# A third buffer for one pair of q and k loads, in the still empty weight slot of the sixth unit, and that unit's rounding three slots later

## The reference

```python
# attention inside chunks of 64 tokens
scores = q_c @ k_c.T / 8
attn = exp(scores - max(scores));  attn = attn / (sum(attn) + 1e-09)
x = (attn @ v_c).reshape(4608, 512)
# first gated network, d_ff = 1536
xn = x / sqrt(mean(x*x) + 1e-06) * rms_g
x = (silu(xn @ w_gate) * (xn @ w_val)) @ w_out
# second network, d_ff = 2048
h = x @ w_in
out = (h * clip(h + 3, 0, 6) / 6) @ w_out2
```

## Time and profile before

| | |
|---|---|
| median of 3 runs | 1652.73 us (1647.89, 1652.73, 1653.22) |
| the profiled execution's own time | 1651.29 us |
| its span, first to last instruction | 1649.5 us |
| mean granted clock of TensorE | 0.996 |
| PE busy | 1605.6 us, 97% |
| DVE, ACT, POOL busy | 64%, 52%, 48% |
| large DMA queue (q1), share of 16 engines | 64.3% |

### The profile page before, as it was taken

How to read it: one execution, slowest core, us unless ns; L and a number is a source line. 1 busy time by engine, 2 the same in 40 slices (tenths; PEclk the granted TensorE clock), 3 DMA queues, 4 the chain that set the end, 5 groups by cost and what they waited for, 6 DMA issues and landing times.

```text
span 1649.5 us, 29728 instructions
## 1 busy us (share of the span) xinstructions
PE 1605.6 (97%) x11335; PEld 1569.5 (95%) x11337; DVE 1047.5 (64%) x1441; ACT 858.5 (52%) x1341; POOL 786.9 (48%) x772
## 2 busy tenths in 40 slices
PE   7889999999999999999999999999999999999998
PEld 5678999899999999999999999999999999999998
DVE  4878877868754556655554776665666765455454
ACT  4666766655544444544444665555655644434432
POOL 2543543449786654434340376777676630231231
PEclk9999999999999999999999999999999999999999
DMA  9577777554566555989997856656658986776674
GB/s 177 133 170 184 176 201 173 143 159 155 167 229 208 195 205 184 366 311 310 311 316 275 304 210 238 210 183 246 227 189 274 372 275 204 220 230 210 212 227 119
DMA packets 335646, 366.88 MB, mean 222 GB/s; under 512 B 186256, under 2 KB 299152, under 8 KB 332304
## 3 DMA queue, kind: packets, MB, share of 16 engines
q1 hardware_dynamic: 321584, 334.69, 64.3%
q0 software_dynamic: 8800, 28.85, 5.1%
q10 hardware_dynamic: 5120, 1.44, 0.5%
HBM read 200.80 MB, written 164.10 MB: 221 GB/s over the span
## 4 chain that ended last, share of the span: by engine, by line
PE 85%; DVE 3%; issue 3%; ACT 2%; DMA 2%; POOL 2%; SPq 2%; ACTq 0%; DVEq 0%; POOLq 0%
PE bx L968 14%; PE by L968 14%; PE bx L970 13%; PE by L970 13%; PE bx L969 13%; PE by L969 13%; DMA hl_b<-h_scratch 1%; SPq L568 1%; PE att L937 1%; PE att L946 1%; PE att L895 1%; DMA hl_d<-u_scratch 1%; PE att L918 1%; DVE wr L1511 1%; DVE tx L1498 1%
## 5 line engine op out<-in xcount | busy, mean ns | idle before, releaser
L968 PE MATMUL by<-tx,wr 128*128 128x384 f32 x840 | 286.2, 341 | 2.7 <-ACT vb L1176 1.0
L968 PE MATMUL bx<-tx,wr 128*128 128x384 f32 x840 | 285.8, 340 | 2.7 <-ACT gb L1176 1.2
L970 PE MATMUL bx<-tx,wr 128*128 128x384 f32 x840 | 281.4, 335 | 0.0
L970 PE MATMUL by<-tx,wr 128*128 128x384 f32 x840 | 281.3, 335 | 0.0
L969 PE MATMUL by<-tx,wr 128*128 128x384 f32 x840 | 281.2, 335 | 0.0
L969 PE MATMUL bx<-tx,wr 128*128 128x384 f32 x840 | 281.2, 335 | 0.0
L1549 DVE TENSOR_TENSOR hl_d<-hl_d 128x1536 fp32r<-128x1536 f32 x84 | 146.2, 1774 | 94.0 <-ACT hl_d L1248 93.9
L1867 POOL DMA_DIRECT2D out_dram<-ot x128 | 70.2, 556 | 248.3 <-DVE ot L1572 245.8
L1549 DVE TENSOR_TENSOR hl_b<-hl_b 128x1152 fp32r<-128x1152 f32 x84 | 118.9, 1431 | 106.1 <-ACT hl_b L1248 105.3
L1248 ACT ACTIVATE hl_d<-hl_d 128x1536 fp32r<-128x1536 f32 x84 | 123.3, 1486 | 113.7 <-DMA hl_d<-u_scratch 113.4
L968 PEld LDWEIGHTS by<-tx,wr 128*128 128x128 f32 x840 | 158.0, 188 | 7.2 <-DVE ub L1523 1.9
(11 more groups left out here) (193 smaller groups left out, 3773.3 us busy)
## 6 DMA issues: line engine op xcount, KB each, us to landing
hl_d<-u_scratch SPq DMA_DIRECT2D x84, 768.0 KB, 4.4
hl_b<-h_scratch SPq DMA_DIRECT2D x84, 576.0 KB, 5.7
u_scratch<-ut SPq DMA_DIRECT2D x48, 576.0 KB, 3.7
h_scratch<-ht SPq DMA_DIRECT2D x36, 576.0 KB, 3.6
u_scratch<-ub SPq DMA_DIRECT2D x96, 192.0 KB, 2.8
u_scratch<-ub SPq DMA_DIRECT2D x48, 384.0 KB, 2.5
h_scratch<-vb SPq DMA_DIRECT2D x72, 192.0 KB, 3.5
h_scratch<-vb SPq DMA_DIRECT2D x36, 384.0 KB, 3.1
```

The lines of the kernel that those rows point to most:

```text
L968: pe.matmul(dst, w_hi, m_hi, start=start, stop=False, skip_group_check=not opens)
L970: return pe.matmul(dst, w_lo, m_hi, start=False, stop=stop, skip_group_check=not opens)
```

## The change

Pair 5 (pieces 10 and 11) gets a buffer of its own, `qk_b`, 8192 bytes a partition in the place of `wr` that unit 5's first part takes later. Its load loses its wait. Pair 6 goes into `qk_a` and waits for pair 4's pieces; its DMAs move from slots 19 to 26 to slots 10 to 17. Pair 7 moves from slots 26 to 33 to 27 to 34. Unit 5's rounding moves on ACT from slots 20 and 24 to 23 and 25, its remainders on DVE from 24 and 26 to 25 and 27, and the first rounding now also waits until the pieces of pair 5 are transposed.

```diff
+    qk_b = at("qk_b", [P, 2, 2 * D], F32, W0 + 71680)
...
-    q_loaded = [sem("q_loaded_a"), sem("q_loaded_c")]
-    k_loaded = [sem("k_loaded_a"), sem("k_loaded_c")]
+    q_loaded = [sem("q_loaded_a"), sem("q_loaded_c"), sem("q_loaded_b")]
+    k_loaded = [sem("k_loaded_a"), sem("k_loaded_c"), sem("k_loaded_b")]
...
     def qk_buf(n):
         n2 = n // 2
-        return 1 if n2 >= 7 and n2 % 2 == 1 else 0
+        return 2 if n2 == 5 else n2 % 2
 
     def qk_loads(n):
         n2 = n // 2
-        return (n2 - 5) // 2 if qk_buf(n) == 1 else n2 - 3 if n2 <= 6 else n2 // 2
+        return (n2 // 2 - 1, (n2 - 5) // 2, 1)[qk_buf(n)]
...
-    QK_FIRST = {5: (5, 2), 6: (19, 2), 7: (26, 2), 8: (41, 2)}
+    QK_FIRST = {5: (5, 2), 6: (10, 2), 7: (27, 2), 8: (41, 2)}
...
-    HI_AT = {2: ((0, 3), (0, 4)), 3: ((0, 9), (0, 10)), 4: ((1, 2), (1, 2)), 5: ((1, 6), (1, 10)),
+    HI_AT = {2: ((0, 3), (0, 4)), 3: ((0, 9), (0, 10)), 4: ((1, 2), (1, 2)), 5: ((1, 9), (1, 11)),
...
-    LO_AT = {2: ((0, 6), (0, 6)), 3: ((0, 9), (0, 12)), 4: ((1, 4), (1, 4)), 5: ((1, 10), (1, 12)),
+    LO_AT = {2: ((0, 6), (0, 6)), 3: ((0, 9), (0, 12)), 4: ((1, 4), (1, 4)), 5: ((1, 11), (1, 13)),
...
-                elif part == 0 and n2 >= 5:
-                    sp.wait_ge(q_transposed, n if n2 in (5, 6) else n - 2)
-                    sp.wait_ge(k_transposed, n if n2 in (5, 6) else n - 2)
+                elif part == 0 and n2 >= 6:
+                    sp.wait_ge(q_transposed, n - 2)
+                    sp.wait_ge(k_transposed, n - 2)
...
+            if u == UA2 - 1 and part == 0:
+                act.wait_ge(q_transposed, 12)
+                act.wait_ge(k_transposed, 12)
             act.activation(parts_to(u, part)[:, :, HI], blocks_of(u, part), ACT.Copy).then_inc(w_hi, 1)
```

More of the change, by code:

```diff
@@ L324, in qk_buf @@
         n2 = n // 2
-        return 1 if n2 >= 7 and n2 % 2 == 1 else 0
+        return 2 if n2 == 5 else n2 % 2
     def qk_loads(n):
         n2 = n // 2
-        return (n2 - 5) // 2 if qk_buf(n) == 1 else n2 - 3 if n2 <= 6 else n2 // 2
+        return (n2 // 2 - 1, (n2 - 5) // 2, 1)[qk_buf(n)]
     def qk_of(n):
         which, full = qk_buf(n), 16 * (P // TB) * (CH // TB) * qk_loads(n)
-        return (qk_a, qk_c)[which], n % 2 * D, (q_loaded[which], full), (k_loaded[which], full)
-    QK_FIRST = {5: (5, 2), 6: (19, 2), 7: (26, 2), 8: (41, 2)}
+        return (qk_a, qk_c, qk_b)[which], n % 2 * D, (q_loaded[which], full), (k_loaded[which], full)
+    QK_FIRST = {5: (5, 2), 6: (10, 2), 7: (27, 2), 8: (41, 2)}
     def qk_slots(n2):
@@ L548, in load_qk @@
             t, p = tp_of(n)
-            buf, which = (qk_a, qk_c)[qk_buf(n)], qk_buf(n)
+            buf, which = (qk_a, qk_c, qk_b)[qk_buf(n)], qk_buf(n)
             for part in parts:
```

## The result

The changed kernel takes 1646.26 us in the median of 14 runs (1641.73 to 1650.68), the kernel before 1652.36 (14 runs, 1647.89 to 1655.28): a ratio of 0.9965, 95% interval 0.9955 to 0.9975, so 0.35% or 5.8 us faster, with an interval of 4.1 to 7.4 us. The forecast was 1647.0, in a range of 1642.5 to 1652.0.

A forecast was written before the change was run, and what follows sets the result against it. PE was taken as the bound, with only its stops in the first three steps, 7.94 us, to win. Terms 1.1 + 1.42 + 0.9 + 0.9 = 4.3 us off 1651.29 gave 1647.0 us, range 1642.5 to 1652.0.

The forecast's parts named there:

- what is late next: Ahead of transpose_x of 9: POOL's chain starts 1.1 us earlier, PE wins 1.1 us, a stop of 1.5 to 2 stays.
- DVE gives less back: Rival, chance 0.25: DVE is the bound, moved remainder eats its cover, store brings nothing; gain 2.5 us, 1648.8 us.
- nothing to be seen: Rival, chance 0.08: pair 5's and pair 6's DMAs crowd each other, loads hidden or late as before; 1651.3 us.
- The slower one: Rival, chance 0.05: unit 5 comes too late, PE stands at slots 29 and 31; 1653.9 us, 2.6 slower.
- All stops go: Rival, chance 0.12: raw weights land earlier, piece 13's exponential is no limit; gain 7.9 us, 1643.4 us.
- my own case: Main forecast, chance 0.50: stops in the first three steps shrink, piece 13's exponential limits; gain 4.3 us, 1647.0 us.
- Pair 5 without a wait: SP's queue: pair 5's last issue at 79.2 to 80.4 us, removing DVE's 1.66 us idle and PE's 0.69 stop.
- Unit 5 three slots later: DVE's moved first remainder (1.34 us) stays covered with 0.6 us to spare; otherwise the price is up to 1.34.
- Scores 12: Pair 6 at slots 10 to 17 removes DVE's 3.28 us idle and PE's whole 1.42 stop; sum by here 2.5.
- The stop of 3.44: Ahead of attend 12: falls to a few tenths, some 2.5 us of new stop at piece 13's transposition; gain 0.9.
- The store behind it: x's store issued 4 to 5 us earlier; DVE's remainder falls from 1.89 to 0.95 us; gain taken 0.9.

The follow-up runs named there:

- e_round_late: The kernel before with only unit 5's later rounding and remainders and pair 7 from slot 27, two buffers as before: ratio 0.9994 to the kernel before.
- e_pair6_waits: The changed kernel with pair 6 back at slots 19 to 26, waiting until pair 5's pieces are transposed: ratio 0.9980 to the kernel before, median 1648.68 us.
- e_pair5_waits: The changed kernel with pair 5's load again waiting for pair 4's transpositions, though its buffer is free: ratio 1.0022 to the kernel before.
- e_round_early: The changed kernel with unit 5's rounding at slots 22 and 24 on ACT, remainders at 24 and 26 on DVE: ratio 0.9963 to the kernel before.
- e_fill_later: The changed kernel with the second operand of step 3 rounded two slots later, at slots 40 and 41: ratio 0.9965 to the kernel before.
- e_fill_later_before: The kernel before with the second operand of step 3 rounded two slots later, the same edit as e_fill_later: ratio 1.0000 to the kernel before.
- r_before: The kernel before run once more, unaltered: ratio 1.0008 to the kernel before.
- e_both: The changed kernel with pair 6 at slots 16 to 23 and step 3's second operand rounded at slots 40 and 41: ratio 0.9958 to the kernel before.
- r_after2: The changed kernel run a third time, unaltered: ratio 0.9963 to the kernel before, median 1645.70 us.

## Why the prediction was right, and where its terms were off

**Direction, range and mechanism held.** SP's wait for qkT vanished, DVE has no idle time for k, PE never waited for `wr` at slots 29 and 31, and a new stop stands ahead of piece 13's transposition. One sign that I had named as a sign of being wrong did appear: the stop ahead of transpose_x of 9 was gone in the first profile and 0.5 to 0.6 us in the repeats, and not 1.5 to 2. So the step "what is late next" was wrong in size; it is the second point below.

Of the rivals, "DVE gives less back" (2.5 us) and "nothing to be seen" are out by the ratio. For the latter I had asked whether loads would crowd each other; they landed as before, v 3.5 us after its issue (median), the raw weights of `in_moe_w_val_dram` 3.7, k of pair 5 2.6, and only its q took longer, 3.2 for 2.6. The slower one is out because PE never stopped for `wr`, and e_round_late has the same time as before. "All stops go" had the five old stops right and not its reasons: the raw weights went out hardly earlier (16.4 us after scores 8, against 16.75), and the exponential of piece 13 was a limit, as my own case had it.

The closeness of the number, 1647.0 against 1646.26, is in part luck. I took the 4.3 us off the profiled execution, 1651.29; off the median of the 14 runs, 1652.36, they give 1648.1, and the medians lie 6.1 apart. The sum for the stretch was 4.3 us; the first two profiles have 4.1, the means of all repeats 114.0 - 109.2 = 4.8. Inside it the terms missed in both directions.

- *Pair 5 without a wait.* Held: its last issues began at 75.80 and ended at 76.8, earlier than the 79.2 to 80.4 that I gave them. e_pair6_waits and e_pair5_waits show its share, and that pair 6 depends on it, which I had not priced.
- *What is late next.* The term was too small: 1.1 us, with a stop of 1.5 to 2 us left ahead of transpose_x of 9. That stop was gone. Relative to scores 8 the instruction came 2.2 us earlier (98.23 - 67.71 = 30.52, now 28.33), and 1.5 and 1.6 in the repeats. The head of POOL's chain moved by 1.3, near the 1.1 that I had, from 89.89 to this:

```profile
86.58 0.73 POOL L1769 TENSOR_TENSOR w_sum_a<-w_raw_a 128x256 f32<-128x256 f32 x1 [2.10 <-DMA w_raw_a<-in_moe_w_val_dram]
...
92.59 0.55 POOL L1862 TENSOR_TENSOR inv_rms<-mean_sq,minus_half 128x1 f32<-128x1 f32 x1
```

  The other microsecond is the inverse root, 0.55 for 1.54. In the repeats the head moved by 0.5 and 0.7 only, since it waited for the raw weights to land (87.54 and 87.28, after scores 8 at 65.90 and 65.76), and there the inverse root is the larger part. The rows for it stood in my own step: I quoted that POOL and DVE slow each other, and used it for step 3's remainder and in the slower rival, not for what the change takes off POOL.
- *Unit 5 three slots later.* The cover held and PE never waited. I had it at nothing in the sum, with a price of up to 1.34 us if the cover failed. It was a gain of 1 us on POOL's chain (e_round_late) and of 1.2 in the stretch (e_round_early, one profile), and nothing that the time shows.
- *Scores 12.* The 1.42 went; the sum by there was 2.5, and it is 42.70 - 39.14 = 3.6, or 2.9 to 3.0 in the two repeats.
- *The stop of 3.44.* Its new limit was named rightly, and e_fill_later confirms it. I expected 2.5 us of stop ahead of that transposition and it was 1.69, with another 0.57 a slot ahead of it. The clock was missing. In three of four profiles in which PE stood for 3.1 us or more ahead of attend 12 it fell to half afterwards; of the four, those with the fall took 23.3 to 25.1 us from scores 12 to 14, the one without 22.40. Of the six profiles with the stop of 1.6 to 1.7 us, in one it fell, the changed kernel's first:

```profile
122.00:124.00 2.00, 0.87 (x5) 0.88 (x6) 2.00 (x2) 1.99 (x4) 1.10 (x1) 0.83 0.70 109
124.00:126.00 2.00, 2.00 (x8) 1.91 (x8) 2.00 (x4) 2.00 (x5) 0.00 (x0) 0.50 0.77 180
126.00:128.00 2.00, 2.00 (x19) 1.75 (x21) 1.61 (x4) 1.12 (x3) 0.00 (x0) 0.82 0.83 129
```

  There 13 to 14 took 11.30 us against 9.91 and 9.38. So a stop can cost its own length and then some slow matmuls: from scores 12 to 14, between profiles of one and the same kernel with the fall and without, 24.21 against 22.40 before and 23.04 against 21.7 after, 1.8 and 1.4 us. A fall need not show in the stretch: in e_round_late the clock was at half from 112 to 114 us, the stop ahead of attend 12 was 1.25 in place of 3.44, and the stretch took 113.25, no more than in my reference profile.

  Whether the clock also makes up the difference between the 4.8 us of the stretch and the 5.8 of the time is not shown. The means of the stretch hold one fall on either side. Against e_fill_later_before, which has a fall too, the changed kernel would gain 6.7, against e_round_late 4.1, and the interval of the measured gain, 4.1 to 7.4 us, holds all of these and 4.8 too. How often each kernel falls over many runs was not counted.
- *The store behind it.* This is the term that is not borne out. The parts seem to come as told: POOL's third sum waited 1.27 us and not 4.06, and the remainder took 0.91 and not 1.89:

```profile
118.99 1.83 POOL L1813 TENSOR_TENSOR xr<-xr 128x768 f32<-128x768 f32 x1 [1.27 <-DMA x_scratch<-xr]
```

```profile
124.65 0.91 DVE L1502 TENSOR_TENSOR tx<-xt,tx 128x768 fp32r<-128x768 f32 x1
```

  But the kernel before has the same 0.91 in its second profile, with the store as late as ever (POOL waited 3.92 us for it), and what had gone from the remainder stood in an instruction ahead of it. DVE of r_before:

```profile
127.92 2.01 DVE L1544 TENSOR_TENSOR vb<-vb,gb 128x384 f32<-128x384 f32 x1
...
131.06 0.91 DVE L1498 TENSOR_TENSOR tx<-xt,tx 128x768 fp32r<-128x768 f32 x1
```

  and of the changed kernel:

```profile
121.75 1.76 DVE L1548 TENSOR_TENSOR vb<-vb,gb 128x384 f32<-128x384 f32 x1
```

  That instruction takes 0.55 us alone. POOL's next sum (`xt_a`, 127.65 to 129.51 in r_before, 121.29 to 123.09 in the changed kernel) so slows one DVE instruction or another, with or without the early store. The 0.9 us as a gain of its own is not shown: r_before has the same time from scores 14 to 19, 47.71 us, as the repeats of the changed kernel (47.66, 47.67). The 0.9 in the sum was made up by the terms ahead of it, 3.6 or 2.9 to 3.0 where I had 2.5.

## What to carry to other kernels

When a DMA queue's wait is taken away, follow the queue and not the buffer: the longest stop was for a v load that stood behind the waiting load, the price of e_pair5_waits came through raw weights behind it, and putting the next load forward paid only once the one before it was out of the way. Cost a moved instruction also by what runs beside it at the old and the new place, since here that turned a feared price into a gain on POOL's chain. And measure between two instructions around the change when the span scatters by more than the change is worth; here three profiles of the changed kernel agree within 0.3 us there and two of the kernel before within 1.2, where the spans of one kernel differed by 7. What such a stretch shows still has to show in the time: e_both and e_round_early moved the one by 1.6 and 1.2 us and not the other.

## What the runs showed of the hardware

**The clock.** The granted clock fell to half after a stop of PE of 3.1 to 3.2 us ahead of attend 12 in three profiles and did not after one of 3.44 in the fourth. Ahead of the transposition of piece 7's probabilities, near 58 to 60 us, PE stands for 3.0 to 3.6 us in every kernel, and there the clock fell in all thirteen profiles. After the stop of 1.6 to 1.7 us ahead of piece 13's transposition it fell in one profile and in five it did not. It also fell after 1.81 us in e_round_late and after 1.23 and 1.96 us close together in e_pair5_waits, and did not after 2.17 in e_fill_later_before (ahead of scores 12) and 2.35 in e_round_early. So the length of the stop alone doesn't tell.

**POOL beside DVE.** POOL's subtraction of 128x384 took 1.01 us alone and 1.97 beside a DVE remainder, and DVE's remainder 1.53 where 1.22 is its usual time: both engines pay. The rows say how much. Whichever starts second is longer by nearly what the first still has to run:

| second to start | alone, us | here | longer by | the other still ran for |
|---|---|---|---|---|
| e_round_early: POOL, 128x384, at 92.64 | 1.01 | 1.97 | 0.96 | 1.12 |
| before: POOL, inverse root, at 95.88 | 0.55 | 1.54 | 0.99 | 1.13 |
| before: DVE remainder at 130.77 | 0.95 | 1.89 | 0.94 | 1.07 |
| after: DVE L1548 at 121.75 | 0.55 | 1.76 | 1.21 | 1.34 |
| r_before: DVE L1544 at 127.92 | 0.55 | 2.01 | 1.46 | 1.59 |

In each of the five the last two columns differ by 0.13 to 0.16 us. An overlap of 0.3 us with the end of an inverse root left a DVE instruction at its usual 0.55 (r_after2, at 122.39). That the second waits for the first to end is a reading of these rows and was not tried by itself. The rule that I cited from the Trainium skill ("GPSIMD Engine Reference", 1. Specifications) agrees with this, and accounts for the one-element inverse root too, 0.55 us alone in e_round_late and 1.54 beside the remainder.
